# The bilinear stage's two input products computed by Strassen's scheme with seven half-size products

## What is computed

```python
x = attention(q, k, v, p)                       # 8 batches, 8 heads, 576 tokens
xn = x / rms(x) * g
y = (silu(xn @ w_gate) * (xn @ w_val)) @ w_o    # 512 -> 1536 -> 512
a = y @ w1                                      # 512 -> 1024
b = y @ w2                                      # 512 -> 1024
out = (a * b @ w3) @ w_out                      # 1024 -> 1024 -> 512
```

## Time and profile before

| | us |
|---|---|
| median of 3 runs | 1400.85 (1398.83 to 1402.58) |
| the profiled execution | 1398.78 |
| its span in the profile | 1397.0 |
| PE busy | 1386.6 |
| DVE busy | 605.9 |
| ACT busy | 407.0 |
| POOL busy | 139.7 |

### The profile page before, as it was taken

The page is one execution under the profiler, slowest core; times in us unless marked ns, Lnnn a source line. Parts: engine busy times, 40 slices in busy tenths (PEclk is TensorE's granted clock), DMA queues, the critical chain, the costliest instruction groups (busy, mean ns, idle before and its releaser), DMA issues.

```text
span 1397.0 us, 22668 instructions
## 1 busy us (share of the span) xinstructions
PE 1386.6 (99%) x9704; PEld 1196.4 (86%) x9704; DVE 605.9 (43%) x1095; ACT 407.0 (29%) x803; POOL 139.7 (10%) x137
## 2 busy tenths in 40 slices
PE   9999999999999999999999999999999999999999
PEld 6699898898998998988989988888888888888887
DVE  4667565565565565655755632221212121212111
ACT  5352433423424334234232422111111111111111
POOL 0100001001000010010012031020202020202000
PEclk9999999999999999999999999999999999999999
DMA  9693633424515425242024130101101010100000
GB/s 325 225 344 86 198 105 90 170 86 130 160 40 175 135 75 187 86 130 78 18 87 151 48 108 1 61 0 61 31 30 61 0 61 1 61 0 31 0 31 30
DMA packets 59364, 129.14 MB, mean 92 GB/s; under 512 B 3712, under 2 KB 12928, under 8 KB 57472
## 3 DMA queue, kind: packets, MB, share of 16 engines
q1 hardware_dynamic: 59264, 127.70, 28.1%
HBM read 106.69 MB, written 20.99 MB: 91 GB/s over the span
## 4 chain that ended last, share of the span: by engine, by line
PE 95%; DVE 2%; ACT 1%; issue 1%; DMA 1%; SPq 0%; DVEq 0%
PE psum L619 9%; PE psum L618 9%; PE psum L620 9%; PE psum L580 8%; PE psum L599 7%; PE psum L581 7%; PE psum L582 7%; PE psum L601 7%; PE psum L600 7%; PE psum L639 5%; PE psum L640 5%; PE psum L638 5%; PE psum L544 4%; PE psum L528 1%; PE psum L507 1%
## 5 line engine op out<-in xcount | busy, mean ns | idle before, releaser
L580 PE MATMUL psum<-a_hi,m_hi 128*128 128x288 f32 x768 | 240.2, 313 | 0.3
L599 PE MATMUL psum<-g_hh,wo_hi 128*128 128x288 f32 x768 | 227.3, 296 | 3.4 <-DVE g_res L963 2.6
L1058 DVE TENSOR_TENSOR b_h<-b_s,psum 128x512 f32<-128x512 f32 x72 | 49.5, 688 | 409.0 <-PE psum L620 409.0
L581 PE MATMUL psum<-a_lo,m_hi 128*128 128x288 f32 x768 | 226.4, 295 | 0.0
L582 PE MATMUL psum<-a_hi,m_lo 128*128 128x288 f32 x768 | 226.1, 294 | 0.0
L601 PE MATMUL psum<-g_hh,wo_lo 128*128 128x288 f32 x768 | 226.0, 294 | 0.0
L600 PE MATMUL psum<-g_hl,wo_hi 128*128 128x288 f32 x768 | 225.9, 294 | 0.0
L618 PE MATMUL psum<-xh,w_hi 128*128 128x512 f32 x576 | 224.1, 389 | 0.0
L619 PE MATMUL psum<-xl,w_hi 128*128 128x512 f32 x576 | 224.1, 389 | 0.0
L620 PE MATMUL psum<-xh,w_lo 128*128 128x512 f32 x576 | 224.1, 389 | 0.0
L580 PEld LDWEIGHTS psum<-a_hi,m_hi 128*128 128x128 f32 x768 | 144.0, 187 | 50.3 <-issue 45.3
(11 more groups left out here) (111 smaller groups left out, 1738.8 us busy)
## 6 DMA issues: line engine op xcount, KB each, us to landing
w_in<-in_w_gate SPq DMA_DIRECT2D x24, 1024.0 KB, 5.4
w_in<-in_w_val SPq DMA_DIRECT2D x24, 1024.0 KB, 5.6
kT<-in_kT SPq DMA_DIRECT2D x8, 1152.0 KB, 7.9
v_sb<-in_v SPq DMA_DIRECT2D x8, 1152.0 KB, 7.3
qT<-in_qT SPq DMA_DIRECT2D x16, 576.0 KB, 3.8
y_scratch<-g_res SPq DMA_DIRECT2D x16, 576.0 KB, 3.1
x_raw<-y_scratch SPq DMA_DIRECT2D x9, 1024.0 KB, 7.7
out<-b_res SPq DMA_DIRECT2D x8, 1024.0 KB, 5.1
```

The costliest lines, as they stand in the source:

```text
L580: nc.tensor.matmul(in_ps[which], hi, a2_hi[:, t, par, :], start=par == 0, stop=False)
L581: nc.tensor.matmul(in_ps[which], hi, a2_lo[:, t, par, :], start=False, stop=False)
L599: nc.tensor.matmul(out_ps[m], hi, hh[:], start=f == 0, stop=False)
```

## The change

`into2` is replaced. The activations of a tile are cut into quarters by contraction half and token half (2 x 128 rows and 256 tokens each), and `w1` and `w2` into quarters by contraction half and output chunk, taken in pairs of 256 output columns (`PAIRS` = 4 for each tile, 36 groups in all). Each group has seven products `P1` to `P7` of half size, each of `w1` and of `w2`, in place of eight. A product is 2 weights x 2 contraction chunks x 3 passes = 12 matmuls with 256 moving columns. Its two halves share one PSUM bank, and four banks (6, 7, 0, 1) go round.

- The sums of weight quarters are made by POOL (`sum_w12`, 4 additions of 128 x 512 for each of 4 pairs), after which ACT and DVE split seven operands of 128 x 512 for each pair.
- The sums of activation quarters are made by POOL (`sum_x`, 4 additions of 128 x 512 for each tile). The split of the activations goes from POOL to ACT and DVE: seven units for each tile, into single buffers `xo_hi` and `xo_lo`.
- The seven products are put together by DVE: seven additions of 128 x 512 with one operand in PSUM (`u2`, `u3`, `c21`, `c22` into `u3`, `u4` into `u2`, `c11` into `e1`, `c12` into `u2`). ACT copies only `P1` out. Four multiplications of 128 x 256 then give the product of the two halves, `h2`, and its split is done with 128 x 512 for each of two chunks.
- Weights come in 16 DMAs of 256 KB, and activations in 4 DMAs of 256 KB for each tile. The first two pairs' weights and the first tile's activations are split in the last 19 slots of the last batch (from slot (0,5)), the others in the first groups (`pair_units`). Slots (0,5) to (1,11) of the last batch have 7 units of `w` pair 0, 7 of `x`, and 5 of `w` pair 1.
- `outof2` keeps its 24 matmuls for two chunks. It stands after `P7` of the next group.

```diff
@@ sums on POOL, behind the eight batches' work @@
+            def sum_w12(p):
+                lo = w_raw[p]
+                pool.wait_ge(w_loaded[p], 16 * 4)
+                nc.gpsimd.tensor_tensor(lo[:, P5], lo[:, P7], lo[:, P4], ALU.add).then_inc(w_sum_ready, 1)
...
+            def sum_x(t):
...
+                nc.gpsimd.tensor_tensor(b12, b22, b12, ALU.subtract).then_inc(x_sum_ready, 1)
...
+                if t:
+                    pool.wait_ge(prod_done[P4], PAIRS * t)
+                nc.gpsimd.tensor_tensor(lo[:, P4], b21, t2, ALU.subtract).then_inc(x_sum_ready, 1)
...
-            for t in range(TILES2):
-                split_x(t)
+            sum_w12(0)
+            sum_x(0)
+            for p in range(1, PAIRS):
+                sum_w12(p)
+            for t in range(1, TILES2):
+                sum_x(t)
@@ PE @@
+                if i == P7 and g:
+                    pe.wait_ge(c11_ready, g)
...
                 for which in range(2):
+                    dst = in2_ps(g, i)[:, which, :]
+                    for c in range(2):
+                        hi, lo = w_hi[p][:, i, which, c, :], w_lo[p][:, i, which, c, :]
+                        nc.tensor.matmul(dst, hi, xo_hi[:, i, c, :], start=c == 0, stop=False)
+                        nc.tensor.matmul(dst, hi, xo_lo[:, i, c, :], start=False, stop=False)
+                        last = nc.tensor.matmul(dst, lo, xo_hi[:, i, c, :], start=False, stop=c == 1)
...
+            def outof2(g):
+                t, p = divmod(g, PAIRS)
+                for f in (1, 0):
+                    pe.wait_ge(hl2_ready[f], g + 1)
...
+            for g in range(GROUPS):
+                for i in range(Q):
+                    product(g, i)
+                    if i == P7:
+                        if g:
+                            outof2(g - 1)
+                        else:
+                            outof(LAST - 1)
+            outof2(GROUPS - 1)
@@ ACT, the last batch's slots @@
-                        if b == B - 1 and t == 1 and 1 <= f <= 2 * KC:
-                            act.wait_ge(w12_loaded[(f - 1) // KC], 16)
-                            nc.scalar.copy(w12_hi[:, f - 1, :], w12_raw[:, f - 1, :]).then_inc(w12_hi_ready, 1)
+                        if b == B - 1 and FC * t + f >= FIRST_UNIT:
+                            unit(UNITS[FC * t + f - FIRST_UNIT])
+                if kind == "w":
+                    act.wait_ge(w_sum_ready, 4 * (a + 1))
+                    nc.scalar.copy(w_hi[a][:, i], w_raw[a][:, i]).then_inc(w_hi_ready, 1)
```

More of the change, by code:

```diff
@@ L30 @@
 TILES2 = B * S // TILE2
+TH = TILE2 // 2
+PAIRS = FC2 // 2
+GROUPS = TILES2 * PAIRS
+Q = 7
+P1, P6, P7, P4, P5, P2, P3 = range(Q)
 SCALE = float(DH) ** -0.5
@@ L49 @@
 WO_LOADS = [slice(0, 1), slice(1, 4), slice(4, 8), slice(8, 12)]
+X_ORDER = (P1, P7, P6, P4, P5, P2, P3)
+UNITS = [("w", 0, i) for i in range(Q)] + [("x", 0, i) for i in X_ORDER] + [("w", 1, i) for i in range(Q)]
+FIRST_UNIT = 5
+LEFT = UNITS[2 * FC - FIRST_UNIT:]
+X_SUM = {P7: 1, P6: 2, P4: 3, P5: 4}
 W_BUFS = 4
@@ L131, in build, with raw_and_lo @@
             a2T = at("a2T", [P, 2, 2, HALF])
[L132 to L136, removed]
-            with ExitStack() as st:
[L138 to L141, removed]
+        w_raw, w_lo, w_hi = [None] * PAIRS, [None] * PAIRS, [None] * PAIRS
+        def raw_and_lo(stack, name, shape):
+            with ExitStack() as st:
+                raw = alloc(st)(f"{name}_raw", shape)
+            return raw, alloc(stack)(f"{name}_lo", shape, F32R)
+        with ExitStack() as st:
+            at = alloc(st)
+            for p in range(2):
+                w_raw[p], w_lo[p] = raw_and_lo(st, f"w{p}", [P, Q, 2, 2, P])
+                w_hi[p] = at(f"w{p}_hi", [P, Q, 2, 2, P], F32R)
+            xo_raw, xo_lo = raw_and_lo(st, "xo", [P, Q, 2, TH])
+            xo_hi = at("xo_hi", [P, Q, 2, TH], F32R)
+            x11, x12 = at("x11", [P, 2, TH]), at("x12", [P, 2, TH])
         const("first_region", [P, 22784])
@@ new lines, in _ @@
+            for g in range(GROUPS):
+                t, p = divmod(g, PAIRS)
+                gap, late = pair_units(g)
+                dve.wait_ge(prod_done[P6], g + 1)
+                dve.wait_ge(e1_out, g + 1)
+                if g:
+                    dve.wait_ge(h12_ready, g)
+                nc.vector.tensor_tensor(u2[:], e1[:], in2_ps(g, P6), ALU.add).then_inc(u2_ready, 1)
+                dve.wait_ge(prod_done[P7], g + 1)
+                dve.wait_ge(u2_ready, g + 1)
+                if g:
+                    dve.wait_ge(h22_ready, g)
+                nc.vector.tensor_tensor(u3[:], u2[:], in2_ps(g, P7), ALU.add).then_inc(u3_ready, 1)
+                for u in gap:
+                    unit(u)
+                if g == 0:
@@ L1069, in _ @@
+                for u in late[3]:
+                    unit(u)
             evict2(TILES2 - 1)
```

343 lines of the change are left out of this document (225 added, 118 removed).

## The result

The changed kernel takes **1375.02 us** (median of 4 runs, 1373.51 to 1377.3) against 1400.10 us for the kernel before in the same comparison (4 runs, 1398.83 to 1402.58): a ratio of 0.982, 95% interval 0.98 to 0.984. The forecast was 1377.0 us, with 1369 to 1391 as range. Profiled against profiled it is 1374.86 against 1398.78 us, 23.9 us less, which is what the sum of the prediction said.

The account below looks back on a forecast made before the run. PE, starting matmuls without a gap in the bilinear stage, was taken as the bound. Savings of 28.8 and 1.5 us less costs of 0.9, 4 and 1.5 gave 23.9 us saved: median 1377.0 us, range 1369 to 1391.

Parts of the forecast that it names:

- The products: Bilinear stage: 1728 matmuls of 226.7 ns become 3024 of 120.0 ns, saving 28.8 us.
- The groups: Bilinear stage: 15.5 us of PE work a group, DVE 7.9 us, no stall in an ordinary group.
- The second rival: In each tile's last group POOL's sums collide with DVE's SBUF work: 1.5 us lost in 8 tiles, 1389 us; chance 0.14.
- The tail: At the very end nothing hides the last group, so PE waits about 0.9 us for the low part.
- The slots: Last batch: the first unit waits for POOL's sums, which also slow DVE's SBUF instructions; cost 4 us, between 0 and 8.
- `w12`: Last batch: without `w12` chunks, the eleven slots from 765.98 to 802.66 us give 1.5 us back.
- Group 0: First group of the bilinear stage: POOL's four weight sums delay DVE's low parts, costing 1.5 us, between 0 and 3.
- The sum: Whole kernel: 28.8 less 0.9, plus 1.5, less 4, less 1.5 = 23.9 us saved; profiled execution 1374.9 us.
- The first rival: Product matmuls: a weight load of 128 columns holds PE for 133.3 ns, however few columns follow; 1417 us, slower; chance 0.10.
- No cost beside the products: Slots and first groups stay clear, so the kernel takes 1371.5 us; chance 0.10.

Follow-up runs that it names:

- the kernel with ten additions: Changed kernel with ten more VectorE additions of 128 x 256 in each group ahead of `c11`, from tile 1 on: 1433.79 us (one run).
- the second profile: The changed kernel as it is, run and profiled again: 1375.22 us, ratio 0.9829.
- the version in step with the slots: Changed kernel with the first unit in slot (0,6) and POOL's eight sums for tile 0 and pair 1 each waiting for one slot's tanh: 1370.21 us.

## Why the prediction was right

*The products.* 3024 matmuls at 120.0 ns were forecast from the line through 288 and 512 columns, and 120.0 were measured. This term carries the result, and it was exact.

*The groups.* Forecast were 15.5 us and no stall in an ordinary group; measured 15.54 and none. Over four groups PE waits for nothing, and low parts end 3.7 us ahead of PE (3.3 forecast). In a tile's last group the first low part ends at 1054.56 and PE wants it at 1056.91: 2.35 to spare, 1.8 forecast. **The second rival**, collisions in every tile, occurs, but once for each tile and not three times, and for half the price. Timeline of DVE of the changed kernel, beside POOL's sum from 1048.59 to 1049.88 us:

```profile
1049.20 0.96 DVE L1254 TENSOR_TENSOR h_raw<-c 128x256 f32<-128x256 f32 x1
```

It takes 0.42 us elsewhere, so the hit is 0.54 us, and the same row comes back in each of the eight tiles. The 2.35 us to spare are what is left behind it. Three hits of 1.1 us would have gone beyond the spare time by about 0.4 us, and the kernel with ten additions shows that PE then waits in every group.

*The tail.* Forecast 0.9 us. PE's last P3 matmul starts at 1363.27, and `outof2` of the last chunk pair at 1364.05 with this row of the changed kernel's timeline; less one distance of 0.12 the stall is 0.66 us; the next matmul starts 0.34 us behind it in place of 0.23, which makes it 0.8 us.

```profile
1364.05 0.50 PE L762 MATMUL psum<-wf_hi,hh 128*128 128x512 f32 x1 [0.50 <-DVE h_lo L1274]
```

*The slots.* Forecast 4 us, measured 3.96; `w12` forecast 1.5, measured 1.34; both together 2.5 against 2.62. The sum was right, its inner split less so: I let PE bear 1.4 us of the wait and had 1.1 left for it, and the rest for collisions. Moving the unit showed that the cover of 1.2 us is shared, and that without the wait only 1.74 us of collisions remain.

*Group 0.* Forecast 1.5 us, measured 0.5 in one profile and nothing in the other: this was the term most off. POOL's sums for the last pair ran at 819.7 to 825.8 us, 4 us later than I had put them, so only two of the low parts ahead of `outof2` at 823.33 were hit, and one in the second profile.

*The sum.* In the stage 28.8 - 0.8 - 0.5 = 27.5 us would be saved, and 26.9 are measured. The 0.6 to 0.7 us between are groups of 15.54 in place of 15.52 us (84 x 0.120 + 24 x 0.2267): each changes its width twice, which costs the 20 ns that the starts around `outof2` show. The prediction had no term for it. An error of 1.0 us in group 0 and one of 0.7 in the groups nearly cancel. That the profiled execution came out within 0.1 us of 1374.9 is thus partly luck, since 1 to 2 us of a run are not the kernel's.

**The first rival**, a floor under the distance, is right in that there is one; it lies at 112 ns in place of 133.3, and it would have decided the result from 128 ns on. The clue taken for it, six transposes 110 ns apart, comes near it, but their weights are 96 columns wide, and whether it is the same floor no run shows. I weighed the rival at 0.10 by the argument that the line would bend only if the floor began exactly at 288; that spoke against 133.3 and not against a floor at 256 columns, and the line does bend, between 192 and 256. That 256 columns still lay 8 ns above the floor was in no row of the kernel before: there the exact 120.0 ns had some luck too.

**No cost beside the products**, 1371.5 us, was not this kernel; but the version in step with the slots is it: 1370.21 us.

## What to carry to other kernels

Where PE runs without gaps, price a restructuring by count times distance, from rows of two widths, and look at the narrowest shape in the trace for a hint of the floor: here halving the width still paid, but one halving more would bring 8 ns a matmul. Work handed to an idle POOL is not free if DVE has operands in SBUF at the same time; put it beside DVE's reads of PSUM, or where DVE waits. A cover counts once: two delays that each fit under it don't fit together.

## What the runs showed of the hardware that I had not expected

- Matmuls of this kind with their own 128-column weight load stand 112 ns apart with 128 and with 192 columns, 120.0 with 256, 133.3 with 288 and 226.7 with 512. So the 13.3 ns above one column a cycle hold from 256 on.
- Joining two matmuls does not bring the 13.3 ns: 512 and 256 columns in turn take 353 ns a pair, 6.7 more than the two in rows of their own, with the operand in one run or in two. A change of width costs in the changed kernel as well, 20 ns there and back around each `outof2`.
- A DVE instruction with both operands in SBUF takes 0.9 to 1.1 us longer beside POOL's sums (0.46 to 1.36 and 1.46, 0.69 to 1.76), and POOL's go from 1.29 to 1.5 and 1.73. With one operand in PSUM it stays at 0.44, and beside a fill of POOL a subtraction of two SBUF operands stays at 0.69. The Trainium skill (SBUF — State Buffer, Who interferes with whom) says just this of two SBUF inputs against one, and the trace agrees.
